# Router logits with the turned tile stationary and the gate matrices moving

## What is computed

```python
# x: (1536, 320), w_gate and w_noise: (320, 8), noise: (1536, 8)
logits = x @ w_gate
noise_scale = np.log1p(np.exp(x @ w_noise))
noisy_logits = logits + noise_scale * noise
top2 = np.argpartition(-noisy_logits, 2, axis=1)[:, :2]
...
for e in range(E):                  # E = 8 experts
    h = np.maximum(x[mask] @ w1[e], 0.0)
    out[mask] += top2_w[mask, k, None] * (h @ w2[e])
```

## Time and profile before

| | |
|---|---|
| median of 3 runs | 735.81 us (734.17 to 736.21) |
| the profiled execution, its own time | 737.39 us |
| its span in the trace | 735.6 us |
| PE busy | 675.1 us, 92% of the span |
| DVE busy | 399.7 us, 54% |
| ACT busy | 286.7 us, 39% |
| POOL busy | 100.6 us, 14% |
| mean granted clock of TensorE | 0.968 of full |

### The profile page before, as it was taken

One profiled execution on the slowest core, in us unless ns is written; L12 is line 12 of the kernel. 1 busy time (PEld: TensorE's weight loads), 2 busy tenths in 40 slices (PEclk: granted clock), 3 DMA queues, 4 the chain that ended last, 5 costly groups with the idle time before them and its releaser, 6 DMA issues.

```text
span 735.6 us, 11126 instructions
## 1 busy us (share of the span) xinstructions
PE 675.1 (92%) x4064; PEld 613.4 (83%) x4065; DVE 399.7 (54%) x667; ACT 286.7 (39%) x470; POOL 100.6 (14%) x138
## 2 busy tenths in 40 slices
PE   2999967899999999899279999999999999999997
PEld 2898825799899899899278999898898888988896
DVE  7577668756545455455246546546544554454422
ACT  6644530455444454454134334333333342332311
POOL 5343301430120220200331000201200001000000
PEclk9999886999999999999779999999999999999999
DMA  8566662376545457940276234344352333422001
GB/s 219 138 145 153 186 176 81 106 213 166 161 133 157 137 163 222 354 130 0 83 226 169 76 102 126 98 127 122 108 154 60 100 114 107 130 85 73 0 0 36
DMA packets 32855, 94.44 MB, mean 128 GB/s; under 512 B 4880, under 2 KB 14864, under 8 KB 32816
## 3 DMA queue, kind: packets, MB, share of 16 engines
q1 hardware_dynamic: 25328, 77.54, 36.4%
q0 software_dynamic: 3264, 11.15, 5.3%
q10 hardware_dynamic: 4224, 5.24, 2.0%
HBM read 79.49 MB, written 14.42 MB: 128 GB/s over the span
## 4 chain that ended last, share of the span: by engine, by line
PE 85%; DVE 6%; issue 4%; DMA 1%; ACT 1%; ACTq 0%; POOL 0%; DVEq 0%; POOLq 0%
PE pY L1148 12%; PE pY L1150 12%; PE pY L1149 12%; PE pH L1133 9%; PE pH L1134 8%; PE pH L1135 8%; PE pH L1138 4%; PE pH L1140 4%; PE psS L977 3%; PE psYa L1030 3%; PE pT L1110 2%; PE psYa L1043 1%; PE psF L1064 1%; PE pH L1092 1%; DVE h_lo L849 1%
## 5 line engine op out<-in xcount | busy, mean ns | idle before, releaser
L577 ACT ACTIVATE h_hi<-pH 128x512 fp32r<-128x512 f32 x160 | 95.7, 598 | 280.4 <-PE pH L1140 275.5
L849 DVE SCALAR_TENSOR_TENSOR h_lo<-pH,h_hi 128x512 fp32r<-128x512 f32 x160 | 110.5, 691 | 166.1 <-ACT h_hi L577 162.1
L1148 PE MATMUL pY<-w_hi,h_hi 128*128 128x320 f32 x608 | 189.9, 312 | 6.1 <-DVE h_lo L849 5.7
L1150 PE MATMUL pY<-w_hi,h_lo 128*128 128x320 f32 x608 | 187.9, 309 | 0.0
L1149 PE MATMUL pY<-w_lo,h_hi 128*128 128x320 f32 x608 | 187.8, 309 | 0.0
L1133 PE MATMUL pH<-x_hi,w_hi 128*128 128x512 f32 (+3 forms) x324 | 124.1, 383 | 8.2 <-issue 5.7
L1148 PEld LDWEIGHTS pY<-w_hi,h_hi 128*128 128x128 f32 x608 | 114.3, 188 | 15.0 <-issue 10.3
L1134 PE MATMUL pH<-x_lo,w_hi 128*128 128x512 f32 (+3 forms) x324 | 121.3, 374 | 0.0
L685 DVE TENSOR_TENSOR w_lo<-stage,w_hi 128x1024 fp32r<-128x1024 f32 (+1 forms) x79 | 107.1, 1356 | 25.4 <-ACT w_hi L523 24.4
L1135 PE MATMUL pH<-x_hi,w_lo 128*128 128x512 f32 (+3 forms) x324 | 120.8, 373 | 0.0
L1149 PEld LDWEIGHTS pY<-w_lo,h_hi 128*128 128x128 f32 x608 | 114.3, 188 | 3.1
(11 more groups left out here) (222 smaller groups left out, 633.2 us busy)
## 6 DMA issues: line engine op xcount, KB each, us to landing
stage<-in_w SPq DMA_DIRECT2D x40, 640.0 KB, 4.0
stage<-in_w SPq DMA_DIRECT2D x40, 512.0 KB, 3.6
stage<-in_w SPq DMA_DIRECT2D x40, 256.0 KB, 3.8
results_by_slot<-acc ACTq DMA_DIRECT2D x8, 640.0 KB, 3.5
results_by_slot<-X SPq DMA_DIRECT2D x8, 640.0 KB
qk<-in_qk_t SPq DMA_DIRECT2D x16, 240.0 KB
kv<-in_kv_n SPq DMA_DIRECT2D x8, 480.0 KB
og<-in_o_n SPq DMA_DIRECT2D x2, 960.0 KB, 9.1
```

The costliest lines, as they stand in the source:

```text
L577: act.activation(HH[s % 2][:, :], pH[s % 2][:, :], ACT.Relu).then_inc(hh_done[layer], 1)
L849: dve.scalar_tensor_tensor(out=HL[s % 2][:, :], in0=pH[s % 2][:, :], scalar=0.0, in1=f32(HH[s % 2][:, :]), op0=ALU.max, op1=ALU.subtract). ...
L1148: pe.matmul(y[:, 0:XD], hh, wh, start=(f == 0), stop=False)
L1150: return pe.matmul(y[:, 0:XD], hl, wh, start=False, stop=(f == NF - 1))
```

## The change

The logits are made tile by tile. The turned tile (`xT`, 128 features by 128 tokens) is now the stationary operand, and `gw` (16 columns) moves. The result has tokens on the partitions and goes straight to the tile's 16 columns of `psL`. With it go `flat`, ACT's three copies to it, PE's twelve transposes back and two semaphores. The third block now uses all 128 rows, so POOL sets rows 0 to 63 of `gw`'s third block to zero, early on. PE makes the logits of tile t-2 behind the transposes of tile t.

```diff
@@ gpsimd
+            pool.memset(gw[0:HB, 2, :], 0.0).then_inc(consts, 1)
             count_up(bases[:, 0:E1 * NT:NT], [[SPAN // P, E1]])
@@ scalar
                 act.activation(xT[:, :, t * P:(t + 1) * P], psT[t % 4][...], ACT.Copy).then_inc(rt_odd, 1)
-                if t % RB == RB - 1:
-                    b = t // RB
-                    act.wait_ge(rt_logit, b + 1)
-                    act.activation(flat[:, b * RB * P:(b + 1) * RB * P], psF[b % 2][0:2 * E1, :], ACT.Copy).then_inc(rt_flat, 1)
-            act.wait_ge(rt_logit_t, 1)
+            act.wait_ge(rt_logit, 1)
             act.activation(ez[:, :, :], psL[:, :, E1:2 * E1], ACT.Exp).then_inc(rt_exp, 1)
@@ tensor
-            pe.wait_ge(consts, 24)
+            pe.wait_ge(consts, 25)
-            def logits(b):
-                pe.wait_ge(rt_even, (b + 1) * RB // 2)
-                pe.wait_ge(rt_odd, (b + 1) * RB // 2)
+            def logits(t):
+                pe.wait_ge(rt_odd if t % 2 else rt_even, t // 2 + 1)
                 for k in range(3):
-                    n = slice(0, P) if k < 2 else slice(HB, P)
-                    if k == 0 and b >= 2:
-                        pe.wait_ge(rt_flat, b - 1)
-                    ins = pe.matmul(psF[b % 2][0:2 * E1, :], gw[n, k, :], xT[n, k, b * RB * P:(b + 1) * RB * P], start=(k == 0), stop=(k == 2))
-                ins.then_inc(rt_logit, 1)
+                    ins = pe.matmul(psL[:, ORDER[t], :], xT[:, k, t * P:(t + 1) * P], gw[:, k, :], start=(t + k == 0), stop=(k == 2), skip_group_check=True)
+                return ins
...
                 ins.then_inc(rt_tr, 1)
-                if t % RB == 1 and t > RB:
-                    logits(t // RB - 1)
-            logits(NT // RB - 1)
-            for b in range(NT // RB):
-                pe.wait_ge(rt_flat, b + 1)
-                for t in range(b * RB, (b + 1) * RB):
-                    ins = pe.transpose(psL[:, ORDER[t], :], flat[:, t * P:(t + 1) * P], ident[0:2 * E1, 0:2 * E1])
-            ins.then_inc(rt_logit_t, 1)
+                if t >= 2:
+                    logits(t - 2)
+            logits(NT - 2)
+            logits(NT - 1).then_inc(rt_logit, 1)
```

More of the change, by code:

```diff
@@ L50 @@
 ORDER = [*range(0, NT, B), *range(1, NT, B)]
-RB = 4
 INV = 4
@@ L135, in build @@
         c_chain, c_done, y_chain, y_read, x_done = sem("c_chain"), sem("c_done"), sem("y_chain"), sem("y_read"), sem("x_done")
-        rt_tr, rt_even, rt_odd, rt_logit, rt_flat, rt_logit_t = (sem(n) for n in ("rt_tr", "rt_even", "rt_odd", "rt_logit", "rt_flat", "rt_logit_t"))
+        rt_tr, rt_even, rt_odd, rt_logit = (sem(n) for n in ("rt_tr", "rt_even", "rt_odd", "rt_logit"))
         rt_chain, rt_exp, rt_ln, rt_top, rt_e2 = (sem(n) for n in ("rt_chain", "rt_exp", "rt_ln", "rt_top", "rt_e2"))
@@ L205, in build @@
         xT = sb("xT", [P, 3, N], F32, turned)
-        flat = sb("flat", [2 * E1, N], F32, turned)
         turned.close()
```

## The result

The change makes the kernel slower. The median went from 736.01 us (4 runs, 734.17 to 737.41) to 745.40 us (4 runs, 743.21 to 746.25); the ratio is 1.0125 with a 95% interval of 1.0093 to 1.0156, some 9 us. The profiled execution of after took 746.25 us with a span of 744.5, where that of before took 737.39 with a span of 735.6; so 8.9 us are to be found in the traces. The forecast was 743.1, its range 739.0 to 746.0: the median lies inside, 2.3 us above the forecast.

What follows compares the result with a forecast made beforehand. PE's order of work, through the router, was taken to set the end. Router +7.4 us and inversion -0.1, with small bounded terms, net +7.3: profiled 737.39 to 744.7, median 735.81 to 743.1 us; range 739.0 to 746.0.

Steps and rivals of the forecast that it cites:

- Half clock for the whole router: Router: PE's thin 16-column records keep the granted clock at half throughout; leads to 743.1 us, chance 0.79.
- Rival A: Router: clock returns to full at 91.6 as before and stays; L758 moves -0.2 to +0.3, 735.8 us, chance 0.11.
- rival C: Router: full clock from 90.42 and loads of 0.067 us a record; L758 2.8 to 3.0 us earlier, 732.9 us, chance 0.03.
- rival D: Router: clock returns midway, at about 98; half of the loss, 739 to 741 us, chance 0.04.
- The price of a record: Router logits: 0.213 us a record at half clock, from L1043, six records a tile making 1.28 us.
- Rival B: Router logits: records keep 0.11 us although the clock is half; 737.4 us, chance 0.03.
- The round: Router, per tile on PE: 1.28 us of logits plus 0.64 of transposes; eight rounds make 15.36 us.
- Switching between the two kinds: Router on PE: alternating transposes and logits can add up to 0.1 us twelve times, +1.2 at most.
- Which branch ends last: Router's end: PE's branch puts L758 at 113.7, +7.4 us; DVE's branch ends earlier, at 112.6.
- What lies beside it: Beside the router: ACT's copies, SP's weight loads and POOL's memset have slack and cost nothing.
- Inversion: Behind the router, DVE's L794/L795 pairs and PE's rounds: shifted against the clock's changes, -0.1 us, between -0.7 and +0.5.
- A shift of L758 is a shift of the end, nearly one to one: From the router's softplus to the kernel's end: all later work depends on it, so its delay passes on nearly whole.

Runs made afterwards that it cites:

- e1: Changed kernel with gw zero-padded to 128 moving columns instead of 16 in the router's logits; 742.28 us, ratio 1.0078 against before.
- e9: Changed kernel with gw zero-padded to 64 moving columns, plus the 175 more PE instructions of e6; 744.83 us, ratio 1.0094 against before.
- e7: Changed kernel with e1's 128 columns, e4's moved weight splits and e6's added PE instructions; 735.87 us, ratio 1.0008 against before.
- e6: Changed kernel with 175 more PE instructions (87 unused one-column matmuls with loads, one semaphore increment) before the first visit; 741.74 us, ratio 1.0076 against before.
- e5: Kernel before with 81 more PE instructions (40 unused one-column matmuls with loads, one semaphore increment) behind the router; 739.68 us, ratio 1.0070 against before.
- e4: e1 with DVE's four weight splits moved between its copies to xT; 739.70 us, ratio 1.0038 against before.
- e2: Kernel before with 84 PE no-operations that did not reach the built program, so a repeat of before; 735.55 us, ratio 0.9992 against before.
- e10: e7 with two unused 512-column matmuls ahead of the first logits and two added one-column matmuls left out; 736.18 us, ratio 0.9993 against before.
- e11: e10 with POOL's weight split also waiting for DVE's last write to X; 734.75 us, ratio 0.9964 against before.
- e3: Changed kernel with 172 PE no-operations that did not reach the built program, so a repeat of after; 747.73 us, ratio 1.0137 against before.
- e8: Changed kernel with POOL's weight split waiting for DVE's last write to X; 746.42 us (2 runs), ratio 1.0149 against before.

## Why the prediction was right, and where it was not

**Half clock for the whole router: right.** It was half from 88.9 to 126.4, with PE busy without a gap in the router. e1 and e9 show the cause that was named, thin streams behind fresh loads: with the same loads it was the width of the stream that decided. Rival A (the clock back at 91.6) and rival C (full clock) fell with the stretch at 92 to 95; rival D fell with the one at 101 to 104.

**The price of a record: right.** 0.213 us at half clock, as taken from L1043; in e9 a record had that price with 64 columns too, and in e1 and e7 0.11 at full clock (0.67 us for six). Rival B, a price without the clock, is refuted by the round of 1.81 us: by it a round would have been 0.67 + 0.64 = 1.31.

**The round: 6% too long.** 1.92 us was the forecast, 1.81 is in the chain. The term that was mis-sized is the one distance at the head of each group of logits: the first record comes 0.213 us behind the last transpose, but the second only 0.073 behind the first, so part of one load is hidden there (in the row 91.65 the six starts span 1.30 less 0.37, which is four distances of 0.213 and one of 0.073). The second transpose comes 0.247 behind the first. Switching between the two kinds, which the prediction bounded from 0 upwards, so gave 0.11 us back in each round. Together with PE's start (89.68 instead of 90.42) tile 10's copy came at 104.59, where 106.0 was forecast.

**Which branch ends last: right.** PE's, over exp, table load and log: 1.88 us from exp to softplus as forecast, and DVE idle for 0.76. The tail was 5.46 us from the last copy to exp against 5.8 forecast. The router's own loss is 6.4 us where the sum had 7.4.

**X earlier by 0.7: not in the sum.** The clock fell at 88.9 and not at 84.8, as the prediction had allowed for (up to -1.5); 1.67 of the 2.27 us gained on PE went again in X's write beside POOL, an encounter that the prediction had not looked at.

**What lies beside it: right.** None of the steps that were costed at nothing (ACT's copies, SP's loads, POOL's fill) is on the chain through the router of after.

**Inversion: right.** From the softplus to the last x_end the shift goes from 5.62 to 5.44, -0.2 against -0.1 forecast.

**"A shift of L758 is a shift of the end, nearly one to one": the step that failed.** It held up to the last x_end (+5.6 at the softplus, +5.4 there), not for PE's branch into the first visit, which the sum put at nothing. The sum counted the duration of each added instruction and not that PE's program became 81 instructions longer ahead of that branch. It cost 3.0 us in the branch and made the visit start at half clock: the shift grows from 5.4 to 10.0 us by the ninth hidden tile. Later stages gave 1.2 back; where was not followed up. By the timed runs this step is 3.7 us (after against e6, by medians; e5 against before gives 3.6 by medians and 5.2 by the ratio), and the router is the other 5.7 (e6 against before, by medians): together the 9.4. What stays open is a part of the router's 5.7. Its 128 columns gave back 3.1 by medians or 3.5 by ratios (after against e1), although the profiles show the router 5.8 shorter. e4's moved splits returned 2.6 more, but e1's profile has only 0.5 us more than before's from X to the softplus, and the intervals reach 2 us and more to either side. The forecast of +7.3 was 1.0 to 1.8 too high for the router and X and had nothing for the branch; the two errors partly cancelled. That is luck: 7.3 and 3.7 together would have been 746.8, outside the range.

The last point has a part that is read and not shown. That the branch's length depends on the length of the program is shown (0.36 at 1592 instructions, 3.35 at 1673 in after and e5, 0.38 at 1848). That PE stands there because the code at the target isn't loaded is argued from the trace's transfers of instructions, 16 KB each. One follows 1.0 to 1.2 us behind the branch's start in every profile, long or short (at 135.62 in before, at 140.77 in after, where the branch starts at 134.54 and 139.77), so it doesn't tell the two apart. The one ahead does: in the six profiles with the long branch it had begun 16.7 to 16.9 us before the branch (123.02 in after), in the seven with the short one 8.8 to 9.5 us (125.13 in before). No run controlled where such a block of code begins.

## What to carry to other kernels

Turning a matmul round, so that the big operand is loaded and a thin one moves, gained nothing here by its thinness: with 128 stationary columns the records kept their distance whatever moved (0.213 us at half clock with 16, 64 and 82 columns, 0.11 at full clock with 41 and 128), and with streams of 16 TensorE was at half clock for a whole stage while it was 100% busy. Pad the moving side before giving the form up (going from 16 to 128 columns gave 3 us here), and read the granted clock of the stage, not the busy share. After any edit that changes how many instructions an engine has, look at the waits on "issue" and at the engine's branches: 3 us appeared, and went again, by instructions that compute nothing.

## What the runs showed of the hardware that was not expected

- **PE's branch into a loop took 0.36 to 0.39 or 3.33 to 3.67 us**, by the number of instructions ahead of it: short in before, e2, e6, e7, e9, e10, e11; long in after, e1, e3, e4, e5, e8. Every profile, before's too, has a second such branch, 3.3 to 3.9 us at the start of the second layer (3.74 at 353.78 in before), where the chain of before goes through a DMA and not through PE. The Trainium skill ("Advanced Engine Details and Errata", section "Control Flow Timing") gives a compare-and-branch some 0.108 us; no run here shows one that short at this place. Elsewhere in before's trace PE's branches last from 0.07 us up.
- **PE was 100% busy at half clock for 20 us**, in one half-clock stretch (88.9 to 126.4; PE was busy throughout up to 110 and paused behind it). With 16 or 64 moving columns for each load the clock didn't return in the router (e9's, after, e6's); with 128 it did (at 98.8 in e1, at 94.0 in e7).
- **One distance is short at a change from transposes to logits**: at half clock the second record of a group comes 0.073 us behind the first (0.107 with 64 columns in e9), against 0.213 within the group; with 128 columns at full clock (e1) all are 0.11.
- **DVE's two-input write took 2.33 us instead of 0.66** beside POOL's split, and 0.66 again once that was moved. The other side of it, in e11 with the split moved behind X: a DVE weight split of 128x1024 took 3.11 us beside it, where the next such split took 1.21.

```profile
87.46 2.90 POOL L454 TENSOR_TENSOR w_lo<-stage,w_hi 128x1280 fp32r<-128x1280 f32 x1 [7.76 <-ACT w_hi L527]
...
88.33 3.11 DVE L685 TENSOR_TENSOR w_lo<-stage,w_hi 128x1024 fp32r<-128x1024 f32 x1
...
91.83 1.21 DVE L685 TENSOR_TENSOR w_lo<-stage,w_hi 128x1024 fp32r<-128x1024 f32 x1
```
